# An MoE-like pair of layers behind a channel attention, float32 on one core: VectorE's side work in layer 1 goes between a pair's activation and its low part, and the seven-product group takes its three plain products first

## The reference

```python
# q, k, v: (1, 6016, 256); w_in: (256, 2048); w_out: (2048, 256); all float32
qn = q / (np.linalg.norm(q, axis=1, keepdims=True) + 1e-06)
kn = k / (np.linalg.norm(k, axis=1, keepdims=True) + 1e-06)
s = kn.transpose(0, 2, 1) @ qn / tau                    # 256 x 256
a = softmax(s, axis=-1)
x = (v @ a)                                             # 6016 x 256
h = x @ w_in1; y = elu(h) @ w_out1                      # layer 1, ELU with alpha 1
h = y @ w_in2; out = (h * sigmoid(h)) @ w_out2          # layer 2, SiLU
```

## Time and profile before

| what | value |
|---|---|
| median of 3 runs | 1039.12 us (1038.87 to 1039.17) |
| the profiled execution | 1039.91 us; its span is 1038.1 us, 1.8 us lie around it |
| TensorE matmuls busy | 1011.3 us, 97% of the span |
| TensorE weight loads busy | 893.4 us, 86% |
| VectorE busy | 806.8 us, 78% |
| ScalarE busy | 702.1 us, 68% |
| TensorE's granted clock | 1.000 |
| DMA | 109.81 MB, mean 106 GB/s |

### The profile page before, as it was taken

How to read it: one execution, slowest core, us unless ns; L and a number is a source line. 1 busy time by engine, 2 the same in 40 slices (tenths; PEclk the granted TensorE clock), 3 DMA queues, 4 the chain that set the end, 5 groups by cost and what they waited for, 6 DMA issues and landing times.

```text
span 1038.1 us, 14074 instructions
## 1 busy us (share of the span) xinstructions
PE 1011.3 (97%) x5058; PEld 893.4 (86%) x5058; DVE 806.8 (78%) x948; ACT 702.1 (68%) x1091; POOL 10.2 (1%) x11
## 2 busy tenths in 40 slices
PE   9999899999999999999999999999999999999998
PEld 8887787888878888888999888888888888888997
DVE  6768788777887877877787776887887887887886
ACT  6687767677676776777767666656656656656664
POOL 0300000000000000000000000000000000000000
PEclk9999999999999999999999999999999999999999
DMA  9903022130321213112032154335335335334333
GB/s 354 351 16 71 41 67 61 46 92 15 107 58 50 70 37 107 46 49 59 1 122 107 71 217 141 137 109 162 137 109 164 137 106 159 131 105 129 108 92 91
DMA packets 115065, 109.81 MB, mean 106 GB/s; under 512 B 89024, under 2 KB 97216, under 8 KB 112448
## 3 DMA queue, kind: packets, MB, share of 16 engines
q1 hardware_dynamic: 114400, 108.58, 32.7%
q10 hardware_dynamic: 608, 0.49, 0.2%
HBM read 83.23 MB, written 25.82 MB: 105 GB/s over the span
## 4 chain that ended last, share of the span: by engine, by line
PE 49%; DVE 18%; ACT 12%; issue 9%; DVEq 0%; ACTq 0%
PE banks L1320 25%; PE banks L1520 20%; DVE g_raw L1021 4%; ACT g_raw L757 4%; ACT g_raw L752 3%; ACT g_parts L767 3%; PE banks L1434 2%; DVE g_parts L1026 2%; DVE g_raw_forms L1037 2%; DVE g_raw_forms L1040 1%; DVE g_raw_forms L1042 1%; PE banks L1460 1%; ACT g_form_parts L778 1%; DVE g_form_parts L1049 1%; DVE v_transposed L945 1%
## 5 line engine op out<-in xcount | busy, mean ns | idle before, releaser
L1320 PE MATMUL banks<-x_parts,w_in_parts 128*128 128x512 f32 (+1 forms) x1152 | 274.9, 375 | 0.3 <-ACT g_pair L858 0.2
L1320 PE MATMUL banks<-xT_parts,a_w_in 128*128 128x512 f32 (+1 forms) x1152 | 261.1, 376 | 2.9 <-DVE g_raw L1021 2.8
L1320 PEld LDWEIGHTS banks<-xT_parts,a_w_in 128*128 128x128 f32 x1152 | 213.5, 189 | 33.2 <-DVE g_raw L1021 5.3
L1320 PEld LDWEIGHTS banks<-x_parts,w_in_parts 128*128 128x128 f32 x1152 | 215.6, 189 | 29.3 <-ACT g_pair L858 1.8
L1520 PE MATMUL banks<-g_pair_parts,w_forms 128*128 128x512 f32 (+1 forms) x987 | 239.3, 375 | 0.0
L1520 PEld LDWEIGHTS banks<-g_pair_parts,w_forms 128*128 128x128 f32 x987 | 186.5, 189 | 22.1
L858 ACT ACTIVATE g_pair<-banks 128x512 f32<-128x512 f32 (+1 forms) x192 | 112.8, 588 | 133.8 <-PE banks L1320 126.9
L1434 PE MATMUL banks<-g_parts,w_out_parts 128*128 128x512 f32 (+1 forms) x745 | 170.4, 375 | 0.0
L1434 PEld LDWEIGHTS banks<-g_parts,w_out_parts 128*128 128x128 f32 x745 | 139.9, 189 | 16.7 <-DVE g_parts L1026 0.3
L1026 DVE TENSOR_TENSOR g_parts<-g_raw,g_parts 128x1024 fp32r<-128x1024 f32 (+1 forms) x63 | 75.9, 1204 | 79.0 <-ACT g_parts L767 79.0
L1204 DVE TENSOR_TENSOR g_pair_parts<-g_forms,g_pair_parts 128x1024 fp32r<-128x1024 f32 (+1 forms) x96 | 115.1, 1200 | 21.4 <-ACT g_pair_parts L867 21.2
(11 more groups left out here) (112 smaller groups left out, 795.8 us busy)
## 6 DMA issues: line engine op xcount, KB each, us to landing
w_forms<-w_forms SPq DMA_DIRECT2D x48, 896.0 KB, 4.7
y_parts<-y1T_parts SPq DMA_DIRECT2D x10, 1024.0 KB, 4.2
x_parts<-y_parts SPq DMA_DIRECT2D x10, 1024.0 KB, 7.0
w_forms<-w_out_forms SPq DMA_DIRECT2D x8, 896.0 KB, 4.2
early_qk<-q SPq DMA_DIRECT2D x23, 256.0 KB, 7.6
early_qk<-k SPq DMA_DIRECT2D x22, 256.0 KB, 8.0
out<-out_tile SPq DMA_DIRECT2D x40, 128.0 KB, 2.7
v_in<-v SPq DMA_DIRECT2D x36, 128.0 KB, 3.6
```

The lines of the kernel that those rows point to most:

```text
L1320: mm = pe.matmul(dst, lhsT, rhs, start=first and n == 0, stop=last and n == len(todo) - 1)
```

## The change

VectorE's order: in each slot the extras now stand between `one_g` and the low part of the pair, except for slots of a seven-product pair, which get none but tile 0's weights. `y_rows` is cut in two, one row sum ahead of `one_g` of slot 2 and one behind it; `y_sums` and the next tile's `v_transpose` go to slot 0, `y1_lo_of` stays in slot 4 but goes ahead of `normal_lo`, `form_sums` go to slot 6 and `form_lo` to slot 7. The two halves of `vT_lo` go to the ends of slots 2 and 4. ScalarE's high parts move with them (`vT_hi` to slot 0, `form_hi` to slot 7 ahead of `normal_hi`). In tile 0 the transpose goes to slot 1, `vT_lo` to slot 4, the form sums to slots 2, 2, 3, 3, their high parts to slots 4 and 5, their low parts to slots 5 and 6.

Tile 0's output leaves its banks by two copies of ScalarE in slot 2 of tile 1 (`first_y_copy`), and its split reads the copies; before, ScalarE and VectorE read the banks. The copy of two half banks (`one_copy`) waits for `y1_lo` in every tile.

TensorE's order: the seven products run M1, M3, M2 (plain), M5, M7, M6, M4, the wait for the low parts of the sums stands behind the first nine matmuls, and M3, which `rows_free` holds in pair 0, is now the second product.

```diff
-SLOT_ONE_FORMS_SUM, SLOT_ONE_FORMS_HI, SLOT_ONE_FORMS_LO = 5, 6, 7
+SLOTS_ONE_FORMS_SUM, SLOTS_ONE_FORMS_HI, SLOTS_ONE_FORMS_LO = (2, 2, 3, 3), (4, 5), (5, 6)
+SLOT_ZERO_V_TURN, SLOT_ZERO_V_HI, SLOTS_ZERO_V_LO = 1, 2, (4, 4)
-SLOT_FORM_SUM, SLOT_FORM_HI, SLOT_FORM_LO = 0, 2, 6
-SLOT_V_TURN, SLOT_V_HI, SLOT_V_LO = 4, 5, 6
+SLOT_FORM_SUM, SLOT_FORM_HI, SLOT_FORM_LO = 6, 7, 7
+SLOT_V_TURN, SLOT_V_HI, SLOTS_V_LO = 0, 0, (2, 4)
-ONE_PRODUCTS = (M1, M5, M7, M6, M2, M3, M4)
-FIRST_OF_BANK = (M1, M7, M2, M4)
+ONE_PRODUCTS = (M1, M3, M2, M5, M7, M6, M4)
+N_PLAIN_PRODUCTS = 3
+FIRST_OF_BANK = (M1, M3, M7, M4)
...
+            def first_y_copy(ph):
+                for c in range(CB):
+                    if c == 0:
+                        act.wait_ge(y_done, 1)
+                    else:
+                        act.wait_ge(p1_down, PAIRS)
+                    act.activation(y_raw(ph, c), y_banks[c][:, 0:ph.n].rearrange("p (h b m) -> p h m b", h=2, m=4),
+                                   ACT.Copy).then_inc(y0_copy, 1)
...
             def slot_one(ph, k):
                 back = shifted(ph, k, 1, PAIRS)
-                if ph.tile == 1 and k == SLOT_ROWS:
-                    y1_lo_of(ONE[0])
                 if ph.tile > 1 and k == SLOT_ROWS:
-                    y_rows(ph.before)
+                    y_row(ph.before, 0)
                 if back:
                     one_g(*back)
-                    one_pair_parts(*back)
-                for tile in (ph, ph.before):
-                    if tile and tile.wino and k + PAIRS * (tile is not ph) == tile.wino[-1] + SUM_LAG:
-                        y_sums(tile)
-                if ph.tile > 1 and k == SLOT_Y1_LO:
-                    y1_lo_of(ph.before)
-                if k == SLOT_V_TURN and ph.v_next:
-                    v_transpose(*ph.v_next[:2])
-                if k == SLOT_V_LO and ph.v_next:
-                    vT_lo(*ph.v_next)
+                if ph.tile > 1 and k == SLOT_ROWS:
+                    y_row(ph.before, 1)
                 if back and weights_in_slot(*back) is not None:
                     weights_lo(dve, weights_in_slot(*back))
-                if ph.tile == 0 and k == SLOT_ONE_FORMS_SUM:
-                    one_forms_sums()
-                if ph.tile == 0 and k == SLOT_ONE_FORMS_LO:
-                    one_forms_lo()
+                if ph.before and ph.before.wino and k + PAIRS == ph.before.wino[-1] + SUM_LAG:
+                    y_sums(ph.before)
+                if ph.tile and k == SLOT_Y1_LO:
+                    y1_lo_of(ph.before)
+                if ph.tile and ph.v_next and k == SLOT_V_TURN:
+                    v_transpose(*ph.v_next[:2])
                 if form_pair(ph) is not None and k == SLOT_FORM_SUM:
                     form_sums(form_pair(ph))
                 if form_pair(ph) is not None and k == SLOT_FORM_LO:
                     form_lo(form_pair(ph))
+                if back and back[1] in back[0].wino:
+                    one_sums(*back)
+                    one_plain_lo(*back)
+                    one_sums_lo(*back)
+                elif back:
+                    normal_lo(*back)
+                if ph.tile == 0 and k == SLOT_ZERO_V_TURN:
+                    v_transpose(*ph.v_next[:2])
+                for c in range(CB):
+                    if ph.v_next and k == (SLOTS_V_LO if ph.tile else SLOTS_ZERO_V_LO)[c]:
+                        vT_lo(*ph.v_next, c)
+                for n in range(4):
+                    if ph.tile == 0 and k == SLOTS_ONE_FORMS_SUM[n]:
+                        one_forms_sum(n)
+                if ph.tile == 0 and k in SLOTS_ONE_FORMS_LO:
+                    one_forms_lo(SLOTS_ONE_FORMS_LO.index(k))
...
                         one_g(ONE[-1], PAIRS - 1)
-                        one_pair_parts(ONE[-1], PAIRS - 1)
                         y_sums(ONE[-1])
+                        normal_lo(ONE[-1], PAIRS - 1)
...
                     if n == 0:
-                        pe.wait_ge(u_lo, 2 * one_pair(ph, k) + 2)
+                        pe.wait_ge(u_lo, 2 * one_pair(ph, k) + 1)
                         if ph.tile == 1 and k == 0:
                             pe.wait_ge(f1_lo, 2)
+                    if n == N_PLAIN_PRODUCTS * len(PARTS):
+                        pe.wait_ge(u_lo, 2 * one_pair(ph, k) + 2)
```

More of the change, by code:

```diff
@@ L260, in build @@
         m1_copy = sem("one_m_copied")
+        y0_copy = sem("first_y_copied")
         c1_sum = sem("one_c_summed")
@@ L783, in one_copy @@
                 act.wait_ge(p1_down, one_pair(ph, ph.wino[-1]) + 1)
-                if ph.tile >= 2:
-                    act.wait_ge(y1_lo, CB * ph.tile)
+                act.wait_ge(y1_lo, CB * ph.tile)
                 act.activation(y_sum(ph, slice(Y_P1, Y_P5 + 1, Y_P5 - Y_P1)).rearrange("p s (m b) -> p s m b", m=4),
                                bank[4][:, 0:ph.n].rearrange("p (s b m) -> p s m b", s=2, m=4), ACT.Copy).then_inc(m1_copy, 1)
+            def first_y_copy(ph):
[6 more added lines that the diff above has]
+                                   ACT.Copy).then_inc(y0_copy, 1)
             def y1_hi_of(ph):
@@ L800, in y1_hi_of, with one_forms_hi @@
                     act.activation(part, y, ACT.Copy).then_inc(y1_hi, 1)
[L802 to L806, removed]
+            def one_forms_hi(i):
+                act.wait_ge(f1_sum, (2, 4)[i])
+                pair_of_forms = (slice(N1, S3 + 1), slice(S2, S4 + 1))[i]
+                act.activation(forms1[:, pair_of_forms, :, 0, :], form1_raw[:, pair_of_forms, :, 1, :],
+                               ACT.Copy).then_inc(f1_hi, 1)
             def form_hi(k):
@@ L817, in slot_one @@
                 if ph.tile == 1 and k == SLOT_ROWS:
-                    y1_hi_of(ONE[0])
+                    first_y_copy(ONE[0])
                 back = shifted(ph, k, 1, PAIRS)
@@ L823, in slot_one @@
                 relu(ph, k, 0)
+                if form_pair(ph) is not None and k == SLOT_FORM_HI:
+                    form_hi(form_pair(ph))
                 if is_wino:
@@ L830, in slot_one @@
                 exp(ph, k, 1)
-                for tile in (ph, ph.before):
-                    if tile and tile.wino and k + PAIRS * (tile is not ph) == tile.wino[-1] + COPY_LAG:
-                        one_copy(tile)
-                if ph.tile > 1 and k == SLOT_Y1_HI:
+                if ph.wino and k == ph.wino[-1] + COPY_LAG:
+                    one_copy(ph)
+                if ph.tile and k == SLOT_Y1_HI:
                     y1_hi_of(ph.before)
-                if k == SLOT_V_HI and ph.v_next:
+                if ph.v_next and k == (SLOT_V_HI if ph.tile else SLOT_ZERO_V_HI):
                     vT_hi(*ph.v_next)
@@ L839, in slot_one @@
                     weights_hi(act, weights_in_slot(ph, k))
[L840 to L843, removed]
+                if ph.tile == 0 and k in SLOTS_ONE_FORMS_HI:
+                    one_forms_hi(SLOTS_ONE_FORMS_HI.index(k))
             for ph in ONE:
@@ L946, in v_transpose, with vT_lo @@
                               v_in[:, 0:n // BLK, :, :].rearrange("p g c i -> p (g c i)")).then_inc(v_tr, 1)
[L948 to L952, removed]
+            def vT_lo(t, n, dst, c):
+                dve.wait_ge(v_hi, CB * t + c + 1)
+                dve.tensor_tensor(columns_of(dst[:, 1, c, 0:n]), v_t[:, 0:n // BLK, c, :],
+                                  columns_of(dst[:, 0, c, 0:n].bitcast(F32)), ALU.subtract).then_inc(v_lo, 1)
             done = [0]
@@ L1056, in one_sums_lo @@
                                   ALU.subtract).then_inc(u_lo, 1)
[L1058 to L1064, removed]
             def y_sums(ph):
@@ L1081, in y_sums, with y_row @@
                                   ALU.add).then_inc(c1_sum, 1)
-            def y_rows(ph):
+            def y_row(ph, c):
                 n = Y_SUMS * (ph.tile - 1)
[L1086 to L1093, removed]
+                if c == 0:
+                    dve.wait_ge(c1_sum, n + 3)
+                    dve.wait_ge(y_done, ph.tile + 1)
+                else:
+                    dve.wait_ge(p1_down, one_pair(ph, PAIRS - 1) + 1)
+                dve.tensor_tensor(y_raw(ph, c), y_banks[c][:, 0:ph.n].rearrange("p (h b m) -> p h m b", h=2, m=4),
+                                  y_raw(ph, c), ALU.add).then_inc(c1_sum, 1)
             def y1_lo_of(ph):
@@ L1276, in tile @@
                         plain_lo(*back)
-                        y_rows(ONE[-1])
+                        for c in range(CB):
+                            y_row(ONE[-1], c)
                     pair_sums(u, k, 0)
```

40 lines of the change are left out of this document (20 added, 20 removed).

## The result

| | before | after |
|---|---|---|
| median of the runs | 1039.03 us | 1006.63 us |
| lowest to highest | 1038.87 to 1039.17 (4 runs) | 1006.42 to 1007.10 (4 runs) |
| profiled execution: time, span | are from it | 1006.43 us, 1004.6 us |

The changed kernel takes 0.9689 of the time before, with a 95% interval of 0.9672 to 0.9706. The forecast was 1007.5 us.

What follows compares the result with a forecast made beforehand. TensorE was taken as the bound, losing 3.15 us a tile to waits and restarts; removing 32 us from the median of 1039.12 gave 1007.1, and 0.4 left for small gaps made 1007.5 us, range 1005.5 to 1013.

Steps and rivals of the forecast that it cites:

- TensorE's floor and the sum: First down product to layer 2: TensorE's work alone is 469 of 500.94 us, so 32 us are gained.
- The walk: Steady tile followed slot by slot in the new order: at least 1.8 us spare at each TensorE wait, all 3.15 gained.
- The cover of 2.0 us in slot 0: Pair 7's normal_lo ends at 5.8 us after slot 0's up starts; TensorE wants it at 7.77.
- Plain products first: Seven-product groups: split wait buys nothing in a steady tile; its price, the first row sum's bank 1.0 us earlier, is covered.
- Tile 0 and tile 1: Tile 0's work spread to at most about 5.0 us a slot against TensorE's 5.18; tile 1's first_y_copy done in time.
- The cover of `one_g` ahead of `up`: Tile 0, slots 4 to 7: one_g done 1.1 us or more ahead of up, the thinnest cover in the kernel.
- The queues and layer 2's start: Moved v loads and form spills stay hidden; y_sums delays the last normal_lo by at most 1.5 us, costing nothing.
- So 2.36 us of extras sit straight ahead of a chain that is 1.4 late: Pair 4: y1_lo_of and the transpose precede one_g, given as why the sums' low part reaches TensorE late.
- The stops of 1.25 us: VectorE stands still 1.25 us after every normal one_g, while ScalarE turns the pair into its high part.
- another wait behind each one removed: No-effect rival: another wait of the same size stands behind each removed one, leaving 1039 us; chance 0.02.
- a row sum's bank: Bank-wait rival: M3 stands until pair 0's first row sum, 0.6 to 1.1 us in 10 tiles, 1018 us; chance 0.07.
- The slower case: Slot 0: pair 7's low part over 2.0 us later than walked makes TensorE wait each tile, up to 1049; chance 0.03.

Runs made afterwards that it cites:

- e7: Changed kernel with the transpose of slot 0 done four times for tiles 2 to 11, ahead of pair 7's low part: 1026.7 us.
- e1: Changed kernel with TensorE's part undone (old order of the seven products, one wait for all low parts): 1006.63 us.
- e2: Kernel before with TensorE's part alone (plain products first, wait for the sums behind nine matmuls): 1039.44 us, ratio 1.0001.
- e5: Changed kernel with tile 0's form sums back together in slot 5, high parts in slot 6, low parts in slot 7: 1009.11 us.
- e3: Changed kernel with each extra in its new slot but behind the pair's low part, and both row sums ahead of one_g: 1030.11 us.
- e8: Changed kernel with the old slot numbers, each extra except vT_lo still between one_g and the low part: 1007.05 us.
- e6: Changed kernel with the transpose of slot 0 done twice for tiles 2 to 11: 1008.31 us.

## Why the prediction was right, point by point

- **TensorE's floor and the sum** held. The groups measured 2.59 and 2.34 us, and 468.4 to 469 was forecast for the stretch that took 468.70. The 0.4 us left for small gaps was not needed.
- **The walk** held. With `up` of slot 0 at 217.07 as time 0, `normal_lo` of pair 7 ends at 222.65, which is 5.6 (forecast 5.8), and the sums' low parts of pair 0 end at 227.78, which is 10.7 (forecast 10.9). No wait of TensorE is left in layer 1 by the list of its waits. The cover of 2.0 us in slot 0 came out as 2.1 in e7.
- **Plain products first buy nothing in a steady tile**: e1 shows it beside the new order, e2 beside the old.
- **Tile 0 and tile 1**: from the first down product to the first seven-product group it took 46.53 us before and 41.44 after; 5.1 less, as the sum implies. Of it, 1.1 us hang on the form work being spread, and 0.5 more of tile 1 (e5: 42.56 and 41.21 us, against 41.44 and 40.72). The cover of `one_g` ahead of `up`, forecast as 1.1 us or more in slots 4 to 7 of tile 0, is 1.0 at its thinnest (`one_g` of pair 3 ends at 78.39, `up` of slot 5 starts at 79.39). One reading of the prediction is too wide: before, not all of tile 0 has such waits; `up` waits three times there, all after 91 us (0.45, 0.58 and 1.50 us), and once for 0.22 in tile 1.
- **The queues and layer 2's start** cost nothing that shows: layer 2 takes 469.4 us before and after.
- **The median** came out 0.9 us under the forecast: 32.4 us were gained where 32 were forecast, the 0.4 left for small gaps was not used, and the median before is 0.1 lower with its fourth run.
- **The step that failed is one of reading, and it cost the time nothing.** "So 2.36 us of extras sit straight ahead of a chain that is 1.4 late" took TensorE's waits as the loss and the extras' slot as its cause. By that reading, as the expectations of e2 and e3 worked it out, e2 had to give 10 us and e3 nearly all 32. They gave 0 and 9. The pace was set by VectorE and ScalarE, and TensorE's waits were where it showed: taken away in one place, they came back in another. The stops of 1.25 us, which the prediction names beside it, were the loss itself. That filling them would also shorten the round of VectorE and ScalarE was not in the prediction; the time came out because the walk had every queue's order in it and asked of each engine in turn.
- **The rivals** fell. The mechanism of the one given least, another wait behind each one removed, is what e2 shows when TensorE's side alone is changed. In the kernel after, nothing in layer 1 waits for a row sum's bank, and pair 7's low part is in time. The slower case's mechanism is real and its threshold as forecast (e7): what goes beyond the cover, 1.71 us, is lost in every tile, 2.08 us with the small gaps behind it.

No kernel beat the changed one; e1 and e8 can't be told from it.

## What to carry to other kernels

Before you add up the waits of the busiest engine, look whether the engine that reads its results ever waits for it: if it hardly does (ScalarE's relu 0.6 us here, against 46.9 after), the engines behind it set the pace, and the tile's length is to be found in their own queue, as work plus stops. Then look for a stop in which an in-order engine waits for another's answer to its own last instruction, and put independent work that is already there into it: here each was worth 1.4 us a tile, in slot 4 as in slot 6, until TensorE's own time was reached. An order walked, with each queue's durations from rows, gave TensorE's 468.7 us from the first down product to layer 2 to 0.3 us; do it for the old order too. I didn't, and I expect that it would have shown the closed round.

## What the runs showed that I had not expected

- A seven-product matmul takes 0.111 us from start to start with 256 columns (189.31 to 189.64 for three) and with 224, while 448 and 512 columns differ (2.27 and 2.59 for twelve, 0.189 and 0.216 each). So the short ones do not go by their columns. The page TensorE: Matmul & The Clock Gate of the Trainium skill, section Back-to-back issue gap, has a sustained 131 ns at 512 columns beside 216 for a single one. This kernel's long rows of matmuls all take the 216.
- e6's layer 1 is unchanged, yet all its four runs are 1.5 to 2.2 us over the median after (1008.09 to 1008.84). In its profiled execution 1.35 us of it lie in layer 2, whose code it does not touch (470.8 against 469.46), and 0.75 in the head. In layer 2 VectorE stands once for 5 us with no releaser that the profile shows, and at 778.45 and 781.44 us TensorE has two waits, of 0.50 and 0.36 us, that the kernel after hasn't. VectorE in e6:

```profile
767.54 0.69 DVE L1212 TENSOR_TENSOR g_forms<-g_pair,g_forms 128x512 f32<-128x512 f32 x1 [0.96 <-issue]
773.20 2.36 DVE L1217 TENSOR_TENSOR g_pair_parts<-g_forms,g_pair_parts 128x1024 fp32r<-128x1024 f32 x2 [4.96 <-issue]
```

The program is longer by a transpose and a wait in each of ten tiles. Length alone doesn't bring the stop: e7 has three of each, its layer 2 takes 469.46 us as after, and VectorE has no stop without a releaser there. The cause stays open.
